# Two slots of the first expert layer with their second product split: scores there, y in the second layer

## The chip, the cores and the metric

One core of a Trainium2 chip runs the whole program. The metric is the device time of the program in microseconds; the time before is the median of three runs.

## The reference

Three parts in a row, all in f32. A linear attention (4 batches, 8 heads, 768 steps, head size 48) makes x of 3072 tokens by 384. Then two layers with 8 experts each:

```python
# first layer: each token goes to its best expert
logits = xn @ en.T / tau
expert_idx = np.argmax(logits, axis=1)
...
h = np.maximum(x[mask] @ w1[e], 0.0)
out[mask] = gate_w[mask, None] * (h @ w2[e])
# second layer: pairs (token, expert) in falling order of score, 384 tokens for each expert
logits = x @ w_gate
order = np.argsort(-flat)
...
h = np.maximum(x[mask] @ w1[e], 0.0)
out[mask] = h @ w2[e]
```

Both layers widen 384 to 1024 and go back. The second layer cannot begin to assign before it has the scores of all tokens, and it assigns greedily: each of seven phases finds the next expert that fills up.

## The kernel before, in words

The attention sorts its rows of x by expert into `sorted_rows`. The first layer (`first_layer`, from L1257) works through slots of 128 rows of one expert; 27 are used here. In a slot `x_transposes` (L1466) turns x on TensorE, 24 matmuls of 128 columns (L1492) make the hidden layer in `p_h`, ScalarE's relu (L1379) writes `hid_t`, and 8 matmuls of 392 columns (L1503) make `p_o`: 384 columns of y, and 8 of the second layer's scores, since `w2s` carries the product of w2 and the second layer's gate beside w2. VectorE writes the scores (`logits_out`, L1439) and y times the gate (L1457); ScalarE's queue stores y in `y_rows` (L1387). The transposes of the next slot stand in the middle of the second product, ahead of its fifth matmul.

Around this ScalarE computes the norm and the exponential for the gate, with a table load ahead of each (L1366, L1383). VectorE works in the order `scale`, `gate`, `x_evac` of the next slot (L1435), `logits_out`, y. SP loads the w1 of slot i + 1 when the hidden layer of slot i - 1 is done (`load_w1`, L39); GpSimd loads the w2 of an expert when the last slot of the expert before last is done. Slots 0 to 2 are written out, the rest run in a hardware loop of two slots per pass (`loop`, L1280).

The second layer (`second_layer`, from L1529) interleaves phases and experts by an order written out by hand in TensorE's function. In phase 0 TensorE has no expert to work on yet. VectorE makes 31 candidate thresholds and compares all scores with them (`offer`, L1765), TensorE counts (`count`, 31 matmuls, L1937), VectorE looks which threshold fits, TensorE spreads the answer (`digit`, L1944); this runs four times. Then `take`, `total` (L1948), `members`, `rank` (L1953), `rows` and `tables` (L1962) give the table of the expert's tokens, `read_table` tells it, GpSimd gathers the rows of `y_rows` (`get`, L1677) and the first expert's products start (L1983, L1999). Fillers (`keep_busy`, L119) stand where TensorE would otherwise rest from `rank` on. A block of the program ends with a barrier of all engines, so one stands between the two layers.

Of the kernel before, what the change touches and what calls it, by code (L numbers as in the profile page):

```python
# [79 lines left out]
WEIGHTS_AT = 10, 11, 16, 17  # L80
QUAD, HF = 4, FF // 2
# [8 lines left out]
def shared(nc, sb, ps, sem, io, keep):  # L90

    for name, shape, kind in (("ident", [P, P], F32), ("mask", [P, P], F32), ("tri", [P, P], BF16),
# [16 lines left out]
                              ("hid_t", [P, KF, P], F32), ("y_row", [P, 2, HD], F32)):  # L109
# [86 lines left out]
def attention(nc, general, sb, ps, sem, io, keep):  # L196
# [40 lines left out]
    w2t = sb("w2t", [P, QUAD, KD, HF], F32)  # L237
# [779 lines left out]
def attention_any(nc, sb, ps, sem, io, keep):  # L1017
# [15 lines left out]
    s_turn = sem("z_turn")  # L1033
# [208 lines left out]
FIRST = ("init", "expert", "turn", "xt", "xtev", "h", "relu", "o", "y", "lgdone", "gate", "ssq", "root", "arg", "exp")  # L1242
# [14 lines left out]
def first_layer(nc, sb, ps, sem, io, keep):  # L1257
    ident = keep["ident"]
    slot_row, slot_expert, last_slot = (keep[n] for n in ("slot_row", "slot_expert", "last_slot"))
    logits, tokens = keep["placed"]  # L1260
    w1s, w2s, s_w, s_slot, s_pads = (keep[n] for n in ("w1s", "w2s", "s_w", "s_slot", "s_pads"))
# [11 lines left out]
    (s_init, s_expert, s_turn, s_xt, s_xtev, s_h, s_relu, s_o, s_y, s_lgdone, s_gate, s_ssq, s_root, s_arg, s_exp,  # L1273
# [3 lines left out]
    SURE = (NT - AHEAD - 1 + 1) // 2  # L1277
    PAIRS = (SLOTS + AHEAD - 3) // 2

    def loop(eng, body):  # L1280

        for i in range(AHEAD + 1):
            body(i, i % 2, i // 2)
        eng.wait_ge(s_plan, SLOT_STEPS)
        used = eng.value_load(last_slot[0:1, E - 1:E], min_val=NT, max_val=SLOTS + AHEAD)
        with eng.Fori(0, SURE) as j:
            body(2 * j + 3, 1, j + 1)
            body(2 * j + 4, 0, j + 2)

        def further(j):  # L1290


            if j < PAIRS:
                with eng.If(used > 2 * j + 3):
                    body(2 * j + 3, 1, j + 1)
                    body(2 * j + 4, 0, j + 2)
                    further(j + 1)
        further(SURE)
        return eng.snap((used // 2) * 2)
# [5 lines left out]
    def is_slot(i, n):  # L1305
        return isinstance(i, int) and i == n

    with nc.Block() as block:
        @block.sync
        def _(sp):  # L1310
# [11 lines left out]
            last = loop(sp, body)  # L1322
            sp.sem_inc(s_init, 1)
            for k in range(2):
                sp.wait_ge(s_slot[k], 16 + 8 * last)
                sp.sem_inc(s_init, 1)
# [22 lines left out]
        def _(act):  # L1349
# [18 lines left out]
            def body(i, q, turn):  # L1368
# [6 lines left out]
                for g in range(0 if is_slot(i, 0) else 2):  # L1375
# [3 lines left out]
                    act.activation(hid_t[:, half * g:half * (g + 1), :], p_h[g][:, :, :], ACT.Relu).then_inc(s_relu, 1)  # L1379
# [6 lines left out]
                act.wait_ge(s_y, i + 1 + CREDIT)  # L1386
                act.dma_start(io["y_rows"][bass.ds(place(i, shifted) * P, P), :], y_row[:, q, :]).then_inc(s_out[q], 16)  # L1387
# [6 lines left out]
            act.sem_inc(s_init, 1)  # L1394

        @block.vector
        def _(dve):
# [47 lines left out]
            def body(i, q, turn):  # L1445
# [9 lines left out]
                logits_out(i, q)  # L1455
                dve.wait_ge(s_out[q], 16 * turn + CREDIT)
# [8 lines left out]
        def _(pe):  # L1465
# [7 lines left out]
            def body(i, q, turn):  # L1473
# [55 lines left out]
def second_layer(nc, general, sb, ps, sem, io, keep):  # L1529
# [63 lines left out]
    w1s, w2s = keep["w1s"], keep["w2s"]  # L1593

# [35 lines left out]
    s_stored = sem("b_stored", False)  # L1630

# [16 lines left out]
    with nc.Block() as block:  # L1648
# [19 lines left out]
        def _(pool):  # L1668
# [21 lines left out]
            pool.wait_ge(s_stored, 1)  # L1690
            get(0)
# [8 lines left out]
        def _(act):  # L1700
# [15 lines left out]
            act.sem_inc(s_stored, 1)  # L1716
            for i in range(TE):
                x_evac(0, i)
# [207 lines left out]
        def _(pe):  # L1926
# [76 lines left out]

            pe.wait_ge(s_v, HIGH)
# [498 lines left out]
```

## Time and profile before

| what | value |
|---|---|
| three runs, us | 828.15, 829.2, 829.27 |
| profiled execution, us | 820.85 |
| its span, us | 819.1 |
| mean granted TensorE clock in it | 0.984 of 2.4 GHz |
| TensorE busy | 779.0 us, 95% |
| VectorE, ScalarE, GpSimd busy | 53%, 39%, 18% |
| first layer's slots, from the profile | 198 to 484 us |
| first search of the second layer | 486 to 515 us |

Times inside the program are read on the profiled execution's scale, from the first instruction of its span. Busy shares are averages over stages with different limits. In the rows an f32 matmul shows as two records and a bf16 one as one; transposes show as one.

### The profile page before, as it was taken

What the parts mean: (1) busy time and instruction counts of PE and PEld (TensorE: products, weight loads), DVE (VectorE), ACT (ScalarE), POOL (GpSimd) and SP (SyncE); (2) the same over time, 40 slices, a digit from 0 to 9 for tenths busy, and PEclk for the clock granted to TensorE, in tenths of its full rate; (3) what the DMA queues carried; (4) which work ended last, traced back from release to release, by engine and by line L of the source; (5) the groups of instructions that cost most, each with busy time, mean ns of one, the idle gap of its engine ahead of it and who ended that gap; (6) DMA issues with size and microseconds to landing.
All of it is one profiled execution on the core that took longest, in us unless ns stands there. A gap on an engine that the chain in (4) does not pass through costs nothing. (4 is left out here: it accounts for less than half of the span.)

```text
span 819.1 us, 17097 instructions
## 1 busy us (share of the span) xinstructions
PE 779.0 (95%) x6003; PEld 562.7 (69%) x6004; DVE 436.7 (53%) x1194; ACT 322.5 (39%) x818; POOL 149.6 (18%) x151
## 2 busy tenths in 40 slices
PE   8999999997999999999999964899999999999996
PEld 7778777876777788887777854655666565655653
DVE  8989898944332232333323348466757677673000
ACT  4878787853444444444444420112121211112120
POOL 5114343430000000000000000106232240402201
PEclk9999999999999999999999995999999999999999
DMA  8879899625667565667575421332515052446100
GB/s 282 310 262 354 312 352 320 237 74 191 221 258 246 204 201 198 221 230 262 183 267 179 163 77 59 126 128 76 183 39 194 22 192 89 143 150 216 50 10 32
DMA packets 68856, 149.71 MB, mean 183 GB/s; under 512 B 4968, under 2 KB 37104, under 8 KB 68784
## 3 DMA queue, kind: packets, MB, share of 16 engines
q1 hardware_dynamic: 53952, 114.03, 39.2%
q0 software_dynamic: 6912, 23.75, 8.5%
q10 hardware_dynamic: 7920, 10.99, 4.1%
q8 instruction: 43, 0.70, 0.4%
q14 instruction: 29, 0.24, 0.1%
HBM read 130.06 MB, written 18.69 MB: 182 GB/s over the span
## 5 line engine op out<-in xcount | busy, mean ns | idle before, releaser
L1503 PE MATMUL p_o<-w2s,hid_t 128*128 (+1 forms) x432 | 152.7, 497 | 0.0
L1492 PEld LDWEIGHTS p_h<-x_t,w1s 128*128 128x128 f32 x1248 | 143.4, 192 | 7.2
L1492 PE MATMUL p_h<-x_t,w1s 128*128 128x128 f32 x1248 | 143.5, 275 | 0.0
L1983 PE MATMUL p_gh<-g_t,w1s 128*128 128x384 f32 x384 | 132.8, 494 | 0.0
L1999 PE MATMUL p_go<-w2s,g_hid 128*128 128x384 f32 x384 | 131.5, 489 | 0.0
L1503 PEld LDWEIGHTS p_o<-w2s,hid_t 128*128 128x128 f32 x432 | 78.7, 192 | 46.3 <-issue 1.8
L1983 PEld LDWEIGHTS p_gh<-g_t,w1s 128*128 128x128 f32 x384 | 70.0, 190 | 45.7 <-issue 6.1
L1999 PEld LDWEIGHTS p_go<-w2s,g_hid 128*128 128x128 f32 x384 | 70.3, 190 | 42.1
L1379 ACT ACTIVATE hid_t<-p_h 128x512 f32<-128x512 f32 x52 | 31.0, 597 | 155.4 <-PE p_h L1492 146.4
L1722 ACT ACTIVATE g_hid<-p_gh 128x384 f32<-128x384 f32 x64 | 31.4, 490 | 113.0 <-PE p_gh L1983 113.0
L1429 DVE TENSOR_SCALAR col<-col 128x1 f32<-128x1 f32 x27 | 4.1, 154 | 131.2 <-ACT ex L1383 131.2
L1677 POOL DMA_INDIRECT g_in<-y_rows,table x24 | 29.2, 1217 | 244.7 <-DVE table L1842 239.9
L1687 POOL DMA_INDIRECT out<-o_row,table x24 | 44.3, 1846 | 80.4 <-ACT o_row L1710 44.8
L1772 DVE TENSOR_TENSOR reach<-free_best,cand 128x3968 bf16<-128x3968 f32 (+2 forms) x19 | 58.6, 3084 | 0.7
L518 ACT ACTIVATE diag_v<-v_pad,diag 128x48 f32<-128x48 f32 x192 | 48.0, 327 | 0.0
L467 POOL TENSOR_TENSOR r_dec<-kr_t,decays 128x512 f32<-128x512 f32 x24 | 28.6, 1192 | 103.2 <-issue 60.4
L1710 ACT ACTIVATE o_row<-p_go 128x384 f32<-128x384 f32 x24 | 11.8, 490 | 87.7 <-PE p_go L1999 87.7
L1703 ACT ACTIVATE g_t<-p_gx 128x384 f32<-128x384 f32 x22 | 10.8, 490 | 70.5 <-PE p_gx L1970 70.5
L1383 ACT ACT_TABLE_LOAD x27 | 34.6, 1283 | 3.7 <-issue 3.2
L1339 POOL COPY w2s<-w2g 128x64 f32<-128x64 f32 x6 | 1.4, 237 | 185.7 <-PE p_o L1503 185.7
L1834 DVE TENSOR_TENSOR row_is<-row_b,iota_p 128x2048 bf16<-128x2048 bf16 (+1 forms) x16 | 34.9, 2221 | 0.3
L1366 ACT ACT_TABLE_LOAD x27 | 34.6, 1283 | 0.5
(269 smaller groups left out, 1052.2 us busy)
## 6 DMA issues: line engine op xcount, KB each, us to landing
w1s<-in_w SPq DMA_DIRECT2D x28, 1536.0 KB, 6.3
kr_t<-in_kr_t SPq DMA_DIRECT2D x24, 512.0 KB, 5.7
w2t<-in_w_t SPq DMA_DIRECT2D x16, 768.0 KB, 7.9
w1s<-in_w1b SPq DMA_DIRECT2D x8, 1536.0 KB, 6.4
w2s<-in_w2b SPq DMA_DIRECT2D x8, 1536.0 KB, 10.0
w2s<-in_w POOLq DMA_DIRECT2D x12, 768.0 KB, 6.4
w_pad<-in_w_t SPq DMA_DIRECT2D x24, 256.0 KB, 6.0
v_pad<-in_v_pad SPq DMA_DIRECT2D x24, 256.0 KB, 8.2
```

Of the source, the lines that this page charges most:

```text
L518: ins = act.activation(diag_v[:, t % 2, h, :], v_pad[:, q, h, 0:D], ACT.Copy, scale=diag[:, t % 2, h:h + 1])
L1366: act.activation(col[:, q, 0:1], col[:, q, 15:16], ACT.Sqrt).then_inc(s_root, 1)
L1379: act.activation(hid_t[:, half * g:half * (g + 1), :], p_h[g][:, :, :], ACT.Relu).then_inc(s_relu, 1)
L1383: act.activation(ex[:, :], lg[:, q, :], ACT.Exp, bias=col[:, q, 9:10], accum_out=col[:, q, 10:11]).then_inc(s_exp, 1)
L1492: ins = pe.matmul(p_h[g][:, m, :], w1s[:, q, a, f:f + P], x_t[:, q, a, :], start=(a == 0), stop=(a == KD - 1))
L1503: ins = pe.matmul(p_o[:, :], hid_t[:, m, :], w2s[:, bass.ds(half, 1), m, :].rearrange("p o n -> p (o n)"), start=(m == 0), stop=(m == KF - 1))
L1687: pool.indirect_dma_start(out=io["out"][:, :], out_offset=place(1, p, i), in_=o_row[:, p % 2, i, :], in_offset=None).then_inc(s_out[p % 2] ...
L1722: act.activation(hid[:, m, :], p_h[(KF * p + m) % 3][:, :], ACT.Relu).then_inc(s_relu, 1)
L1772: dve.tensor_tensor(reach(n)[:, at, :], free(p)[:, at].unsqueeze(2).broadcast_to([P, len(part), n]), cand[:, 0:n].unsqueeze(1).broadcast_t ...
L1834: dve.tensor_tensor(row_is[:, at, :], row_b[:, 1, at].unsqueeze(2).broadcast_to([P, size, P]), iota_p[:, :].unsqueeze(1).broadcast_to([P, ...
L1983: ins = pe.matmul(p_h[n % 3][:, :], w1s[:, p % 2, a, m * P:(m + 1) * P], x_t[:, a, :], start=(a == 0), stop=(a == KD - 1))
L1999: ins = pe.matmul(p_o[n % 2][:, :], hid[:, m, i * P:(i + 1) * P], w2s[:, p % 2, m, 0:HD], start=(m == 0), stop=(m == KF - 1))
```

## The change

The slots 3 and 4 (`LATE`) are late slots. There the second product takes only the 8 score columns of `w2s`, the next slot's transposes stand ahead of it, the relu writes `hid_late`, VectorE keeps the gate in `gate_late` in place of writing y, and no y is stored. SP loads the late slots' w2 into `w2_late` (room that the attention used for `w2t`), once after the third and once after the sixth pass of its loop. In the second layer's phase 0 TensorE makes the two y's with 16 matmuls of 384 columns (`late`), in groups between the steps of the search; ScalarE multiplies by the gate and stores, and GpSimd's first gather waits for both stores. Six of the ten fillers after `rank` and one between the halves of `tables` go. One more pair of slots is written out, and the loop has one pass less. A semaphore is saved by reusing another (`s_init`, `z_turn`).

```diff
+LATE = AHEAD + 1, AHEAD + 2
...
+                              ("gate_late", [P, len(LATE)], F32)):
         keep[name] = sb(name, shape, kind)
 
...
     wg, w2g = keep["wg"], keep["w2g"]
-    w2t = sb("w2t", [P, QUAD, KD, HF], F32)
...
-    SURE = (NT - AHEAD - 1 + 1) // 2
-    PAIRS = (SLOTS + AHEAD - 3) // 2
+    FIXED = LATE[-1] + 1
+    SURE = (NT - FIXED + 1) // 2
+    PAIRS = (SLOTS + AHEAD - FIXED) // 2
+
+    def loop(eng, body, between=None):
+        for i in range(FIXED):
             body(i, i % 2, i // 2)
...
-        with eng.Fori(0, SURE) as j:
-            body(2 * j + 3, 1, j + 1)
-            body(2 * j + 4, 0, j + 2)
+        parts = [range(0, SURE)] if between is None else [range(0, 3), range(3, 6), range(6, SURE)]
+        for n, part in enumerate(parts):
+            if n > 0:
+                between(n - 1)
+            with eng.Fori(part[0], part[-1] + 1) as j:
+                body(2 * j + FIXED, 1, j + FIXED // 2)
+                body(2 * j + FIXED + 1, 0, j + FIXED // 2 + 1)
...
+
+    def late(i):
+
+        return LATE.index(i) if isinstance(i, int) and i in LATE else None
+
+    def hidden(i):
+        return hid_t if late(i) is None else keep["hid_late"][:, late(i), :, :]
...
-            last = loop(sp, body)
-            sp.sem_inc(s_init, 1)
+
+            def load_late(k):
+                expert = sp.value_load(slot_expert[0:1, LATE[k]:LATE[k] + 1], min_val=0, max_val=E - 1)
+                sp.dma_start(w2_late[:, k, :, :], io["w2"][bass.ds(expert, 1), :, :].rearrange(
+                    "o (m p) n -> p (o m) n", p=P)).then_inc(s_w[k], 16)
+            last = loop(sp, body, load_late)
...
-                    act.activation(hid_t[:, half * g:half * (g + 1), :], p_h[g][:, :, :], ACT.Relu).then_inc(s_relu, 1)
+                    act.activation(hidden(i)[:, half * g:half * (g + 1), :], p_h[g][:, :, :], ACT.Relu).then_inc(s_relu, 1)
...
                 act.wait_ge(s_y, i + 1 + CREDIT)
+                if late(i) is not None:
+                    act.sem_inc(s_out[q], 16)
+                    return
                 act.dma_start(io["y_rows"][bass.ds(place(i, shifted) * P, P), :], y_row[:, q, :]).then_inc(s_out[q], 16)
...
                 logits_out(i, q)
+                if late(i) is not None:
+                    dve.tensor_copy(keep["gate_late"][:, late(i):late(i) + 1], col[:, q, 12:13]).then_inc(s_y, 1)
+                    return
                 dve.wait_ge(s_out[q], 16 * turn + CREDIT)
                 dve.tensor_scalar(y_row[:, q, :], p_o[:, 0:HD], col[:, q, 12:13], None, ALU.mult).then_inc(s_y, 1)
...
-                    if m == 4 and not first:
+                    if m == (4 if late(i) is None else 0) and not first:
                         x_transposes(i + 1, 1 - q, turn if q == 0 else turn + 1)
-                    ins = pe.matmul(p_o[:, :], hid_t[:, m, :],
-                                    w2s[:, bass.ds(half, 1), m, :].rearrange("p o n -> p (o n)"),
+                    of = slice(0 if late(i) is None else HD, HD + E)
+                    ins = pe.matmul(p_o[:, of], hidden(i)[:, m, :],
+                                    w2s[:, bass.ds(half, 1), m, of].rearrange("p o n -> p (o n)"),
                                     start=(m == 0), stop=(m == KF - 1))
                 ins.then_inc(s_o, 1)
...
             pool.wait_ge(s_stored, 1)
+            pool.wait_ge(s_late_stored, 16 * len(LATE))
             get(0)
...
+            shifted = act.value_load(keep["shift"][0:1, 0:1], min_val=0, max_val=AHEAD)
+            for k, i in enumerate(LATE):
+                act.wait_ge(s_late, k + 1)
+                act.activation(y_late[:, k, :], p_o[k][:, :], ACT.Copy, scale=keep["gate_late"][:, k:k + 1]
+                               ).then_inc(s_late_out, 1)
+                act.wait_ge(s_late_out, k + 1)
+                act.dma_start(io["y_rows"][bass.ds((i - shifted) * P, P), :], y_late[:, k, :]
+                              ).then_inc(s_late_stored, 16)
...
+                if p == 0 and i > 0:
+                    pe.wait_ge(s_late_out, i)
...
+            def late(k, blocks):
+
+                for m in blocks:
+                    if m == 0:
+                        pe.wait_ge(keep["s_w"][k], 32)
+                    ins = pe.matmul(p_o[k][:, :], keep["hid_late"][:, k, m, :], w2_late[:, k, m, :],
+                                    start=(m == 0), stop=(m == KF - 1))
+                    if m == KF - 1:
+                        ins.then_inc(s_late, 1)
+
+            late(0, range(0, 1))
             pe.wait_ge(s_v, HIGH)
             pe.transpose(p_m[0:1, :], high[:, :], ident[:, :]).then_inc(s_bound, 1)
             pe.wait_ge(s_v, BOUND)
             pe.matmul(p_m[:, 0:1], ones[0:1, :], bound[0:1, :], start=True, stop=True).then_inc(s_bound, 1)
-            for k in range(len(FAR)):
-                count(0, k)
-                digit(0, k)
+            late(0, range(1, 4))
+            count(0, 0)
+            digit(0, 0)
+            late(0, range(4, 6))
+            count(0, 1)
+            digit(0, 1)
+            late(0, range(6, 8))
+            count(0, 2)
+            digit(0, 2)
+            late(1, range(0, 2))
+            count(0, 3)
+            digit(0, 3)
+            late(1, range(2, 3))
             total(0)
+            late(1, range(3, 5))
             rank(0)
-            keep_busy(pe, 10, p_h[2][:, 0:P], ident)
-            tables(0, 5)
+            late(1, range(5, 8))
+            keep_busy(pe, 4, p_h[2][:, 0:P], ident)
+            tables(0, 4)
             keep_busy(pe, 15, p_h[2][:, 0:P], ident)
             count(1, 0)
```

TensorE in a slot of the first layer, `first_layer`, slot 3. Before (in the loop, the same as slot 2 written out): `p_h` is the hidden layer, `p_turn` the next slot's transposed x, `p_o` y and scores. The ISA rows compute addresses.

```order
L1492 MATMUL p_h<-x_t,w1s 128x128 x24
L1495 REGISTER_ALU
L1503 ISA
L1503 MATMUL p_o<-w2s,hid_t 128x392
...
L1470 MATMUL p_turn<-ident,x_in 128x128 x3
L1503 ISA
L1503 MATMUL p_o<-w2s,hid_t 128x392
```

And now:

```order
L1520 MATMUL p_h<-x_t,w1s 128x128 x24
L1523 REGISTER_ALU
L1498 MATMUL p_turn<-ident,x_in 128x128 x3
L1532 ISA
L1532 MATMUL p_o<-w2s,hid_late 128x8
...
L1507 TENSOR_LOAD slot_expert
```

The second product has 8 columns in place of 392, and the transposes have moved from its middle to its front.

TensorE in the first search of the second layer. Before (`p_search` holds counts and answers, `p_rows` the maximum, ranks and tables, `p_gh` the fillers' target):

```order
L2005 MATMUL p_rows<-ident,high 1x128
L2007 MATMUL p_rows<-bound,ones 128x1
L1937 MATMUL p_search<-takers,reach 31x8 x31
L1944 MATMUL p_search<-hit,ones_bf 128x1
...
L1948 MATMUL p_search<-taken_now,ones_bf 128x248
L1953 MATMUL p_rows<-member,tri 128x31
L1954 MATMUL p_rows<-before,ones_bf 128x31
L122 MATMUL p_gh<-ident 128x128 x10
```

And now:

```order
L2054 MATMUL p_go<-w_late,hid_late 128x384
L2061 MATMUL p_rows<-ident,high 1x128
L2063 MATMUL p_rows<-bound,ones 128x1
L2054 MATMUL p_go<-w_late,hid_late 128x384 x3
L1980 MATMUL p_search<-takers,reach 31x8 x31
L1987 MATMUL p_search<-hit,ones_bf 128x1
L2054 MATMUL p_go<-w_late,hid_late 128x384 x2
...
L1991 MATMUL p_search<-taken_now,ones_bf 128x248
L2054 MATMUL p_go<-w_late,hid_late 128x384 x2
L1996 MATMUL p_rows<-member,tri 128x31
L1997 MATMUL p_rows<-before,ones_bf 128x31
L2054 MATMUL p_go<-w_late,hid_late 128x384 x3
```

One late matmul has come ahead of the maximum, three ahead of the first count, two ahead of each later count, one and two around the total and three behind the rank, where four fillers are left.

## Rows read from the trace of the kernel before

**Rows 1.** Timeline, slot 3: start us, us, engine, line, op, tiles, idle before

```profile
226.19 2.80 PE L1503 MATMUL p_o<-w2s,hid_t 128*128 x8
...
227.00 1.28 ACT L1383 ACT_TABLE_LOAD   x1
...
228.72 0.15 DVE L1429 TENSOR_SCALAR col<-col 128x1 f32<-128x1 f32 x1 [4.90 <-ACT ex L1383]
...
229.74 0.56 DVE L1437 COPY x_t<-p_turn 128x384 f32<-128x384 f32 x1
...
231.78 5.52 PE L1492 MATMUL p_h<-x_t,w1s 128*128 128x128 f32 x48
```

**Rows 2.** Windows: us, then PE, PEld, DVE, ACT, POOL busy, clock, DMA share, GB/s

```profile
491.00:506.00 15.00, 5.80 (x129) 4.40 (x129) 11.57 (x44) 0.00 (x0) 0.00 (x0) 0.50 0.00 1
506.00:511.40 5.40, 3.94 (x23) 3.75 (x23) 4.91 (x14) 0.00 (x0) 0.00 (x0) 0.71 0.50 176
```

**Rows 3.** Windows of one microsecond, PE alone: busy, clock, DMA share, GB/s

```profile
488.00:489.00 1.00, 0.34 (x2) 0.82 0.00 0
...
509.00:510.00 1.00, 1.00 (x9) 0.94 0.72 266
```

**Rows 4.** Timeline, end of the first layer and first search

```profile
481.15 2.80 PE L1503 MATMUL p_o<-w2s,hid_t 128*128 x8
...
486.53 0.42 DVE L1846 SCALAR_TENSOR_TENSOR at_best<-logits 128x248 f32<-128x248 f32 x1 [1.62 <-PEq L1308]
...
488.66 0.58 PE L2007 MATMUL p_rows<-bound,ones 1*128 1x1 f32 x2 [0.94 <-DVE bound L1854]
...
491.18 1.12 PE L1937 MATMUL p_search<-takers,reach 128*31 128x8 bf16 x31 [1.94 <-DVE reach L1772]
...
492.51 0.15 DVE L1780 TENSOR_TENSOR filled<-p_search,room 31x8 f32<-31x8 f32 x1
...
492.91 0.18 PE L1944 MATMUL p_search<-hit,ones_bf 31*128 31x1 bf16 x1 [0.61 <-DVE hit L1781]
...
494.51 1.12 PE L1937 MATMUL p_search<-takers,reach 128*31 128x8 bf16 x31 [1.42 <-DVE reach L1772]
...
503.78 0.60 PE L1948 MATMUL p_search<-taken_now,ones_bf 128*128 128x248 bf16 x1 [1.10 <-DVE taken_now L1788]
...
506.15 0.21 PE L1953 MATMUL p_rows<-member,tri 128*128 128x31 bf16 x1 [1.77 <-DVEq L1888]
```

**Rows 5.** Timeline, from the rank to the first gather

```profile
506.23 3.85 PE L122 MATMUL p_gh<-ident 128*128 128x128 f32 x20
...
507.29 0.39 SPq L1656 DMA_DIRECT2D w1s<-in_w1b  x1
...
513.86 3.59 PE L122 MATMUL p_gh<-ident 128*128 128x128 f32 x30
...
515.44 1.03 POOL L1677 DMA_INDIRECT g_in<-y_rows,table  x1 [101.07 <-DVE table L1842]
```

**Rows 6.** Timeline of PE, short products in the attention

```profile
121.08 0.83 PE L875 MATMUL p_route<-enT,x_tr 128*128 128x8 f32 x6
121.78 0.63 PE L919 MATMUL p_kb<-ident,k_dec 128*128 128x128 f32 x4
```

**Rows 7.** Groups of the page: count, busy us, mean ns, idle before

```profile
L1492 PEld LDWEIGHTS p_h<-x_t,w1s 128*128 128x128 f32 x1248 | 143.4, 192 | 7.2
```

**Rows 8.** Line L1356, the 26 loads of x: from issue to landing

```profile
DMA to landing us min/median/max: 2.3/2.4/5.1
```

**Rows 9.** DMA issues of the page: count, KB each, median us to landing

```profile
w1s<-in_w SPq DMA_DIRECT2D x28, 1536.0 KB, 6.3
```

**Rows 10.** Chain that ended last: start us, us, what (total, second product)

```profile
541.28 0.45 PE p_search L1948
...
581.84 5.16 PE p_go L1999 x16
```

**Rows 11.** Line L1387, the 27 stores of y: from issue to landing

```profile
DMA to landing us min/median/max: 1.8/2.0/7.0
```

More of the change, by code:

```diff
@@ L236, in attention @@
     wg, w2g = keep["wg"], keep["w2g"]
-    w2t = sb("w2t", [P, QUAD, KD, HF], F32)
+    w2t = keep["w2_late"][:, :].rearrange("p (j a f) -> p j a f", j=QUAD, a=KD)
     w2g_t = sb("w2g_t", [P, HF], F32)
@@ L1032, in attention_any @@
     s_k = sem("z_const")
-    s_turn = sem("z_turn")
+    s_turn = keep["first"]["turn"]
     s_in = sem("z_in")
@@ L1239, in route_any @@
     return {"sync": on_sync, "gpsimd": on_gpsimd, "vector": on_vector, "tensor": on_tensor}
-FIRST = ("init", "expert", "turn", "xt", "xtev", "h", "relu", "o", "y", "lgdone", "gate", "ssq", "root", "arg", "exp")
+FIRST = ("expert", "turn", "xt", "xtev", "h", "relu", "o", "y", "lgdone", "gate", "ssq", "root", "arg", "exp")
 FIRST_PAIRS = ("xin", "xfree", "out")
@@ L1260, in first_layer @@
     logits, tokens = keep["placed"]
+    w2_late = keep["w2_late"][:, :].rearrange("p (k m n) -> p k m n", k=len(LATE), m=KF)
     w1s, w2s, s_w, s_slot, s_pads = (keep[n] for n in ("w1s", "w2s", "s_w", "s_slot", "s_pads"))
@@ L1276, in first_layer @@
     SCALE, GATE = 9, 13
-    SURE = (NT - AHEAD - 1 + 1) // 2
-    PAIRS = (SLOTS + AHEAD - 3) // 2
-    def loop(eng, body):
-        for i in range(AHEAD + 1):
+    FIXED = LATE[-1] + 1
[3 more added lines that the diff above has]
+        for i in range(FIXED):
             body(i, i % 2, i // 2)
@@ L1285, in loop @@
         used = eng.value_load(last_slot[0:1, E - 1:E], min_val=NT, max_val=SLOTS + AHEAD)
-        with eng.Fori(0, SURE) as j:
-            body(2 * j + 3, 1, j + 1)
-            body(2 * j + 4, 0, j + 2)
+        parts = [range(0, SURE)] if between is None else [range(0, 3), range(3, 6), range(6, SURE)]
[5 more added lines that the diff above has]
+                body(2 * j + FIXED + 1, 0, j + FIXED // 2 + 1)
         def further(j):
             if j < PAIRS:
-                with eng.If(used > 2 * j + 3):
-                    body(2 * j + 3, 1, j + 1)
-                    body(2 * j + 4, 0, j + 2)
+                with eng.If(used > 2 * j + FIXED):
+                    body(2 * j + FIXED, 1, j + FIXED // 2)
+                    body(2 * j + FIXED + 1, 0, j + FIXED // 2 + 1)
                     further(j + 1)
@@ L1393, in _ @@
             act.wait_ge(s_xin[1], 16 + 8 * last + CREDIT)
-            act.sem_inc(s_init, 1)
+            act.sem_inc(s_turn, 1)
         @block.vector
@@ L1593, in second_layer @@
     w1s, w2s = keep["w1s"], keep["w2s"]
+    y_late = sb("y_late", [P, len(LATE), HD], F32)
+    w2_late = keep["w2_late"][:, :].rearrange("p (k m n) -> p k m n", k=len(LATE), m=KF)
     p_s = ps("p_search", [P, E + 2 + E * SLOTS])
@@ L1630, in second_layer @@
     s_stored = sem("b_stored", False)
+    s_late = sem("b_late", False)
+    s_late_out = sem("b_late_out", False)
+    s_late_stored = sem("b_late_stored", False)
     def rows_out(eng):
```

8 lines of the change are left out of this document (5 added, 3 removed).

## The prediction

> **What bounds the kernel now.** I went from the clock and the windows to the two places that the diff touches, a slot of the first layer and the first search of the second layer, and read each as a timeline. The sums are made against the profiled execution, 819.1 us of span inside 820.85 us. The three plain runs have a median of 829.2 us, 8.35 us more. I take differences from the profile and subtract them from 829.2, which assumes that the extra 8.35 us lie in neither place.
>
> In the first layer TensorE never rests. Slot 3 shows it [rows 1]: its second product begins at 226.19 (8 records are 4 matmuls, since an f32 matmul leaves two records), and the next slot's first product begins at 231.78, 5.59 us later. The same 10.95 or 10.96 us stand between the starts of all slots from the second on. Under that lies a second chain which is hidden today: after the last relu ScalarE loads a table at 227.00, VectorE's gate starts at 228.72, and the copy of the next slot's transposed x, which the next product needs, runs from 229.74 to 230.30 [rows 1].
>
> In the search it is the other way round. TensorE is 5.80 us busy in the 15 us from 491 to 506, at half clock [rows 2], and VectorE's chain sets the time. The granted clock is 0.82 in the microsecond from 488 and 0.94 in the one from 509 [rows 3]. So it falls to 1.2 GHz about 4.9 us after the last product of the first layer (481.15 + 2.80 = 483.95 [rows 4]) and comes back about 3 us after the fillers that start at 506.23 [rows 5].
>
> **Part 1: the late slots, a saving.** Slots 3 and 4 multiply 8 columns of w2s instead of 392. A full matmul costs 5.3 us / 8 = 0.66 there. The nearest short one is the attention's 128x8 product: 6 records from 121.08 to 121.78, 0.233 us for each f32 matmul, bound by its weight loads [rows 6]. So 8 of them take 1.87 us instead of 5.28: TensorE gets 3.4 us per slot. It cannot use all of it. The x copy ends 230.30 - 226.19 = 4.11 us after the second product begins, and with 0.2 us for the signal and one weight load (0.19 [rows 7]) the next product starts at 4.31, not 5.59. That is **1.28 us per slot, 2.56 in all**. The bounds are 0.9 (the short product or the next x is late too) and 3.4 (VectorE's chain doesn't count).
>
> The transposes move from the middle of the second product to its start, 2.6 us earlier. They need the next slot's x, whose load landed in 2.3 to 5.1 us [rows 8]. Even one that comes 1.5 us into the second product ends in front of the gate's last step, so I charge nothing. The multiply of y (VectorE) and the y store (ScalarE's queue) go from these slots; they were beside TensorE's work. Two more slots written out instead of looped cost nothing that the profile shows: slot 2, written out, follows the same period as the looped ones.
>
> **Part 2: two more weight loads.** SP issues 1536 KB twice, each right behind a w1s load of the same size, which lands in 6.3 us [rows 9]. Two in a row land in at most 12.6. The w1s load is first in the queue, and the next one has a full slot and a half (5.6 + 5.4 + 5.6 = 16.6 us from issue to need). Nothing on SP waits behind them but the next w1s load, which is issued a slot later. Charged at nothing; if x's own load is pushed past 5.1 us twice, it could be 0.9 us.
>
> **Part 3: 16 matmuls in the gaps, a cost that hangs on the clock.** A 128x384 matmul takes 5.16 / 8 = 0.645 us at 2.4 GHz [rows 10]. At 1.2 GHz no row shows one. Its bounds are twice that, 1.29, and 1.03, by the fillers, whose 20 records took 3.85 us at the low clock and 30 took 3.59 at the high one, a factor of 1.6 [rows 5]. I take 1.29, because 384 columns outweigh the weight load more than 128 do.
> - The first matmul sits ahead of the transpose of the maximum. VectorE starts at 486.53 after the barrier [rows 4]; TensorE is free at the same time and done near 487.2, when VectorE's maximum is not yet ready. Nothing.
> - Three follow the small product of 488.66 + 0.58 = 489.24. At 2.4 GHz they end at 491.18, exactly where the first count starts: nothing. At 1.2 GHz they end at 493.1.
> - Two stand between an answer (492.91 + 0.18 = 493.09) and the next count (494.51): a gap of 1.42 us for 1.29, the same ahead of the second, third and fourth count. One goes ahead of the total (503.78), two between the total's end at 504.38 and 506.15, a gap of 1.77, and three more take the place of six fillers [rows 4, 5]. All fit at 2.4 GHz.
>
> Which clock? One matmul of 0.65 us in the idle 5 us is little, so I expect the clock to fall as before. But the three dense ones then fill TensorE from 489.24, like the fillers from 506.23 which brought the clock back in 3 us. Until 492.2 they do 3.0 / 1.29 = 2.3 matmuls, the rest takes 0.45 us: 492.7. The count adds 1.1, and VectorE, which went on at 492.51 [rows 4], goes on at 493.8: **1.3 us late**. From there on the clock is full, where it was at half before. The total took 0.60 us at the low clock and 0.45 at the high one [rows 10]; with some 0.1 us of each of the three later counts (an estimate from that pair) I take **0.5 us back**.
>
> One row speaks for the return, the fillers of rows 5; one against it, the search from 491 to 506, in which TensorE worked 5.80 of 15 us and the clock stayed at half throughout [rows 2]. The late matmuls lie between the two. If they act like the fillers the part costs 0.8 us, if like the search 6.2 (the second rival). The Trainium skill (TensorE: Matmul & The Clock Gate, What's actually happening) says that the throttled clock is the default and that activity releases it; by that rule it would be the 0.8, and the trace agrees at the fillers but not in the search.
>
> **Part 4: the late stores.** The gather at 515.44 [rows 5] must now wait for the two late y stores. The last late matmul ends near 506.4 + 1.9 = 508.3; with a ScalarE copy of 0.5 and 0.3 to issue, the store starts at 509.1. y stores landed in 1.8 to 7.0 us, median 2.0 [rows 11]: 510.9 to 516.1. The phase's w1s load, issued at 507.29, shares the engines until about 513.5 [rows 5]. Most likely it is down before 514.6, some 0.8 in front of the gather, where the table is told: nothing, up to 1.5.
>
> **Sum:** -2.56 + 1.3 - 0.5 = -1.8 us, so **827.4 us**.
>
> **Rivals.**
> - *The clock does not fall*, because the first matmul and the three dense ones leave too short a rest (18%). For it: the rest shrinks from over 7 us of near idleness to about 5. Against it: 4.9 us sufficed before. Then the search loses nothing and gains 0.5: 829.2 - 2.6 - 0.5 = 826.1.
> - *The clock falls and stays down through the search* (13%, the slower side). Place: the gaps of phase 0. Then three gaps of 1.42 us hold 2.58, 1.16 late each; the block of three costs 1.75 after VectorE's slack of 0.2; the two behind the total 0.8 and the one ahead of it 0.2: 6.2 us. 829.2 - 2.6 + 6.2 = 832.8. It decides from the point where the clock is still 0.50 at the second count; more than 2.5 us lost is a loss over all. For it: each count and each answer still leaves TensorE idle for some 0.5 us. Against it: with the added matmuls TensorE rests far less than in rows 2.
> - *The late store holds the gather* (10%): 1.5 us on the forecast, 828.9.
> - *The slot follows TensorE alone* (5%): 2 x 3.4 saved, 829.2 - 6.8 + 0.8 = 823.2. Against it the x copy of rows 1.
> - *The first layer gives less than it says* (12%): x or the added loads come late in and around the late slots, 1.3 saved in place of 2.56: 828.7.
>
> **The numbers.** The forecast holds 42%; its own range is 826.5 to 828.9 (the clock back at once, or one stretch later). About 0.2%, 1.66 us, is what a measurement can tell from no change, so faster means under 827.5. That is 0.25 of the forecast's 0.42, the full clock and the TensorE case: 0.48. Slower, over 830.9, is the low clock and 0.02 of late stores: 0.15. The rest is 0.37. The range leaves out the TensorE case and the low clock, together 0.18, and reaches from the full-clock case with its bound to a clock that returns halfway: 825.6 to 830.6.
>
> **What would show it.** In the late slots the next product should start 4.3 us after the second begins, with the idle time ended by the x copy. The layer's last product should end near 481.4 on the profile's scale. In the search: the clock at 0.50 for one stretch of 3 to 5 us and then 1.00, the first count about 1.5 us later against the small product, the later gaps of 1.4 unchanged, and the gather released by the table and not by a store. I am wrong if the search is longer by over 2.5 us, or if a late slot's saving is not near 1.3.

## The result, and the profile after

| what | before | after |
|---|---|---|
| median, us | 828.46 (20 runs) | 832.06 (20 runs) |
| profiled execution, its span, us | 820.85, 819.1 | 829.61, 827.8 |
| mean granted TensorE clock | 0.984 | 0.978 |
| TensorE busy, us | 779.0 | 790.3 |

The ratio after to before is **1.004, 95% interval 1.0029 to 1.0051**: some 3.3 us slower (2.4 to 4.2). I had forecast 827.4 us, faster than before, with a range up to 830.6. The forecast was wrong in direction and in range.

The page of the profile after, its span and busy times:

```profile
span 827.8 us, 17095 instructions
...
PE 790.3 (95%) x6021; PEld 569.9 (69%) x6022; DVE 435.9 (53%) x1194; ACT 323.6 (39%) x820; POOL 145.3 (18%) x151
```

TensorE is busy 11.3 us longer. Some 3 us of that are new work: the two short products (1.85 to 1.98 us each) come on top of the moved columns, and seven fillers go. For the rest the same kind of work takes it longer: that is a first sign of the clock.

**Where the time went, by stages.** A slot's period runs from the start of its first product to that of the next. The first layer is taken from the start of slot 1's first product to the end of its last product, the search from VectorE's first step to the first gather.

| stage, us | before | after |
|---|---|---|
| periods of slots 3, 4, 5 | 10.95, 10.96, 10.96 | 9.57, 11.12, 13.69 |
| first layer | 285.84 | 286.85 |
| search | 28.91 | 31.97 |
| first gather to the second layer's first product | 8.67 | 7.51 |
| second layer's first product to the end | 295.0 | 298.1 |

The three slots lost 1.5 us where 2.56 were to be won, and the search lost 3.1 us. The last row is not laid to the change: over all kernels of this study it lies between 293.2 and 298.8 us, and it was 297.5 in one without a late slot. Nor is the period of slot 1, which is 10.96 to 12.56 us in kernels with and without the change, nor the time ahead of it (slot 1's first product starts at 198.11 before, at 200.78 after, and at 202.68 in e8, a kernel without a late slot), nor the row above the last, 6.97 to 9.04 us. They differ from one profiled execution to the next, so below only slots 3 to 5, the search and the timed ratio are compared.

**The first layer after.** Timeline of TensorE from 219 to 262 us (start, length, engine, line, operation, tiles, idle before; the counterpart of [rows 1]):

```profile
222.97 5.52 PE L1520 MATMUL p_h<-x_t,w1s 128*128 128x128 f32 x48
230.20 0.52 PE L1498 MATMUL p_turn<-ident,x_in 128*128 128x128 f32 x3 [1.72 <-DMA x_in<-sorted_rows]
230.56 1.98 PE L1532 MATMUL p_o<-w2s,hid_late 128*128 x16
232.54 7.02 PE L1520 MATMUL p_h<-x_t,w1s 128*128 128x128 f32 x48
239.41 0.49 PE L1498 MATMUL p_turn<-ident,x_in 128*128 128x128 f32 x3
239.73 1.85 PE L1532 MATMUL p_o<-w2s,hid_late 128*128 x16
243.66 8.25 PE L1520 MATMUL p_h<-x_t,w1s 128*128 128x128 f32 x48 [2.07 <-DVE x_t L1462]
```

Slot 3 is 222.97 to 232.54, slot 4 is 232.54 to 243.66. The short products take 1.98 and 1.85 us, as forecast (1.87). But the first products behind them, the same 48 records, take 7.02 and 8.25 us and not 5.52. The same stretch in windows of one microsecond, TensorE alone (total, busy, granted clock, share and rate of the DMA engines):

```profile
229.00:230.00 1.00, 0.00 (x0) 1.00 0.89 184
...
232.00:233.00 1.00, 0.99 (x6) 0.57 1.00 414
233.00:234.00 1.00, 1.00 (x7) 0.50 1.04 430
...
236.00:237.00 1.00, 1.00 (x11) 1.00 0.81 284
...
242.00:243.00 1.00, 0.00 (x0) 0.69 0.97 385
...
246.00:247.00 1.00, 1.00 (x6) 0.50 0.55 141
...
249.00:250.00 1.00, 1.00 (x10) 0.90 0.00 0
```

In each late slot the engine waits 1.7 or 2.1 us and works 1.9 us on 8-column matmuls, and each time the granted clock falls to 0.50 (1.2 GHz). It is back at 1.00 by 236 in slot 4, some 3 us into the next first product. In slot 5 it comes back only in the microsecond from 249, of which it spends 0.2 at the low clock (0.90): 5.5 us in. That explains the periods: -1.38 in slot 3; +0.16 in slot 4, which is -1.34 and +1.50 (7.02 against 5.52); +2.73 in slot 5 (8.25 against 5.52).

**The search after**, timeline from 490 us on (counterpart of [rows 4]):

```profile
490.24 0.42 DVE L1889 SCALAR_TENSOR_TENSOR at_best<-logits 128x248 f32<-128x248 f32 x1 [1.64 <-PEq L1325]
...
492.36 0.58 PE L2063 MATMUL p_rows<-bound,ones 1*128 1x1 f32 x2 [0.94 <-DVE bound L1897]
...
492.87 4.21 PE L2054 MATMUL p_go<-w_late,hid_late 128*128 128x384 f32 x6
...
497.01 0.99 PE L1980 MATMUL p_search<-takers,reach 128*31 128x8 bf16 x31
...
498.62 2.93 PE L2054 MATMUL p_go<-w_late,hid_late 128*128 128x384 f32 x4
...
501.48 0.96 PE L1980 MATMUL p_search<-takers,reach 128*31 128x8 bf16 x31
...
503.04 1.56 PE L2054 MATMUL p_go<-w_late,hid_late 128*128 128x384 f32 x4
...
504.53 1.09 PE L1980 MATMUL p_search<-takers,reach 128*31 128x8 bf16 x31
```

The three late matmuls take 4.21 us, and the first count starts 4.65 us after the small product, where it was 2.52 before (488.66 to 491.18 [rows 4]): 2.1 us. The next two take 2.93 us, and from the first count to the second there are 4.47 us (497.01 to 501.48) for 3.33 before: 1.1. The two after them take 1.56 us, and from the second count to the third there are 3.05 for 3.22 before: 0.2 back. The stretches behind that are within 0.04 us of those of before.

There is a third fall, outside these rows. In all ten kernels here that have the late matmuls the clock falls once more, in nine of them at the products for the tables, where the change took fillers away: after, TensorE rests 2.11 us ahead of them (1.32 before) and the clock is at 0.50 from 518.9 to 522.3. The gather comes no later by it, since VectorE's steps set its time. But the fillers behind it run longer, and the next phase's first count waits for them.

### The profile page after: what moved, and what is told of

Its sections match the earlier page's. It is cut to its first block and busy times, and to the rows that moved or that the text cites. A ratio compares the mean times of both kernels' runs of the same rounds, so it can differ in the third digit from the quotient of the medians.

```text
span 827.8 us, 17095 instructions
## 1 busy us (share of the span) xinstructions
PE 790.3 (95%) x6021; PEld 569.9 (69%) x6022; DVE 435.9 (53%) x1194; ACT 323.6 (39%) x820; POOL 145.3 (18%) x151
## 3 DMA queue, kind: packets, MB, share of 16 engines
q10 hardware_dynamic: 7920, 10.99, 4.0%
## 5 line engine op out<-in xcount | busy, mean ns | idle before, releaser
L1520 PEld LDWEIGHTS p_h<-x_t,w1s 128*128 128x128 f32 x1248 | 147.3, 196 | 8.9 <-issue 2.2
L1520 PE MATMUL p_h<-x_t,w1s 128*128 128x128 f32 x1248 | 147.8, 280 | 2.1 <-DVE x_t L1462 2.1
L1532 PE MATMUL p_o<-w2s,hid_t 128*128 (+1 forms) x400 | 142.2, 499 | 0.0
L1532 PEld LDWEIGHTS p_o<-w2s,hid_t 128*128 128x128 f32 x400 | 73.5, 194 | 43.3 <-issue 2.4
L1401 ACT ACTIVATE hid_t<-p_h 128x512 f32<-128x512 f32 x48 | 28.7, 597 | 145.5 <-PE p_h L1520 145.5
L1721 POOL DMA_INDIRECT out<-o_row,table x24 | 39.9, 1664 | 79.5 <-ACT o_row L1745 44.5
L481 POOL DMA_INDIRECT sorted_rows<-rows,pos x24 | 30.2, 1259 | 19.2 <-DVE rows L727 11.6
```

Of the source, the lines that this page charges most:

```text
L1520: ins = pe.matmul(p_h[g][:, m, :], w1s[:, q, a, f:f + P], x_t[:, q, a, :], start=(a == 0), stop=(a == KD - 1))
L1532: ins = pe.matmul(p_o[:, of], hidden(i)[:, m, :], w2s[:, bass.ds(half, 1), m, of].rearrange("p o n -> p (o n)"), start=(m == 0), stop=(m = ...
L1721: pool.indirect_dma_start(out=io["out"][:, :], out_offset=place(1, p, i), in_=o_row[:, p % 2, i, :], in_offset=None).then_inc(s_out[p % 2] ...
```

## The experiments

My theory (A in the expectations) was: **the clock makes the whole loss, in both places.** A late slot gives TensorE's time back as idle time, the clock falls, and the next full product pays more than the slot saved; in the search the matmuls run at the low clock. The rivals were that late loads of x or w2, the earlier transposes, or the written-out slots cost it. Each ratio is to runs of the kernel before on the same chip. "Slots" is the sum of the periods of slots 3 to 5, 32.87 us before.

| kernel | slots, us | search, us | ratio, 95% |
|---|---|---|---|
| the change | 34.38 | 31.97 | 1.004, 1.0029 to 1.0051 |
| e0, the change again | 34.92 | 30.68 | 1.0037, 1.0021 to 1.0054 |
| e1, first layer's part alone | 34.81 | 28.91 | 1.0023, 1.0003 to 1.0044 |
| e2, search's part alone | 32.87 | 30.89 | 1.0014, 1.0 to 1.0029 |
| e3, fillers behind the short product | 35.61 | 30.06 | 1.0016, 0.9992 to 1.0041 |
| e4, x copy ahead of the gate | 33.89 | 31.94 | 1.0014, 0.9998 to 1.003 |
| e5, fillers ahead of the transposes | 30.32 | 30.69 | 0.9982, 0.9964 to 1.0 |
| e6, e5 and fillers at the barrier | 30.32 | 28.87 | 0.9937, 0.9918 to 0.9955 |
| e6b, the same again | 30.32 | 28.83 | 0.9955, 0.9933 to 0.9976 |
| e7, e2 and fillers at the barrier | 32.87 | 29.17 | 0.9989, 0.9975 to 1.0002 |
| e8, before with fillers in the search | 32.87 | 30.09 | 1.0007, 0.999 to 1.0024 |
| e9, transposes back in the middle | 34.87 | 31.99 | 1.0032, 1.0018 to 1.0046 |

**First layer alone.** The late slots give their scores; the second layer is as before. The y of two slots is left out.

```diff
-            last = loop(sp, body, load_late)
+            last = loop(sp, body)
...
-            late(0, range(1, 4))
+            for k in range(len(FAR)):
+                count(0, k)
+                digit(0, k)
```

> The first-layer half of the change alone: slots 3 and 4 make only their scores, the second layer is as before, the two w2 loads are left out, and the y rows of the two slots are left out of the computation (a stale y_row is stored in their place). Theory A, the clock falls in the late slots: TensorE's clock drops to 1.2 GHz around slots 4 and 5, the three slots from 3 to 5 take 33 to 35 us instead of 32.9, and the kernel is 0 to 2 us slower than before. Theory B, the loss is all in the search: the slots save 1.28 us each and the kernel is 2.6 us faster.

Timeline of its TensorE:

```profile
231.54 0.52 PE L1495 MATMUL p_turn<-ident,x_in 128*128 128x128 f32 x3 [1.68 <-DMA x_in<-sorted_rows]
...
234.38 8.08 PE L1517 MATMUL p_h<-x_t,w1s 128*128 128x128 f32 x48
...
246.55 7.17 PE L1517 MATMUL p_h<-x_t,w1s 128*128 128x128 f32 x48 [2.07 <-DVE x_t L1459]
```

The two slow first products stand here without any late load of w2, so the added loads do not make them. Nor do the late matmuls: the search is 28.91 us, as before. TensorE has 2 x 3.4 us less to do, and the slots take 1.9 us more.

**Search alone.** Slots 3 and 4 make and store their whole y, and the second layer makes it again.

```diff
-                    if m == (4 if late(i) is None else 0) and not first:
+                    if m == 4 and not first:
...
-                    of = slice(0 if late(i) is None else HD, HD + E)
+                    of = slice(0, HD + E)
```

> The second-layer half alone: slots 3 and 4 make and store their whole y in the first layer as before, and the same y is made once more by the 16 matmuls in the gaps of the search, with both w2 loads and both late stores. Theory A: 2 to 3 us slower than before, from late matmuls at 1.2 GHz ahead of the first two counts; the first layer keeps 10.96 us for each slot. Theory B: over 5 us slower, since this half must hold the whole loss and the 2.6 us that the first layer saves.

The search loses 2.0 us with a first layer that is as before. Slots 3 and 4 are written out here as in the change, their relu writes `hid_late`, and they keep 10.95 and 10.96 us: being written out costs them nothing. The search:

```profile
492.31 3.92 PE L2050 MATMUL p_go<-w_late,hid_late 128*128 128x384 f32 x6
496.16 0.93 PE L1976 MATMUL p_search<-takers,reach 128*31 128x8 bf16 x31
...
497.69 1.56 PE L2050 MATMUL p_go<-w_late,hid_late 128*128 128x384 f32 x4
```

The block of three takes 3.92 us, the next two 1.56: the clock is back one gap earlier than in the profile of the change. The parts' excesses, 0.0023 and 0.0014, add up to the 0.0037 of the change measured again. Their intervals (0.0003 to 0.0044 and 0 to 0.0029) are too wide for that to exclude a third cost; it shows only that none is needed.

> The change as it is, for a second trace on the chip of the three runs beside it. Both theories: 2 to 4 us slower than before. Theory A, the clock falls in the late slots and around the first late matmuls: the first layer from its first looped product to its end takes 1 to 2 us more than before, and the search from VectorE's first step to the first gather 2 to 3 us more than 28.9.

The change again, on the chip of e5 to e9: the slots take 10.07, 12.22 and 12.63 us, the search 30.68. How the loss is shared between the places varies; the timed loss is the same within its interval.

**Fillers behind the short product.** Nine matmuls of the identity follow it.

```diff
                 ins.then_inc(s_o, 1)
+                if late(i) is not None:
+                    keep_busy(pe, 9, p_spare[:, :], ident)
```

> The change with nine fillers of 128x128 behind the short product of each late slot, into a PSUM bank of their own, so that TensorE works until the next x is there. Theory A: the clock stays at 2.4 GHz, slots 3 to 5 take about 30.3 us, and the kernel is 3 to 4 us faster than the change without them. Theory B: no difference, or slower by the fillers' overhang.

```profile
228.00:229.00 1.00, 0.92 (x6) 0.66 0.85 213
```

```profile
228.08 0.67 PE L1499 MATMUL p_turn<-ident,x_in 128*128 128x128 f32 x3 [2.02 <-DMA x_in<-sorted_rows]
...
231.82 3.83 PE L125 MATMUL p_spare<-ident 128*128 128x128 f32 x18
...
242.88 2.25 PE L125 MATMUL p_spare<-ident 128*128 128x128 f32 x18
245.10 5.62 PE L1521 MATMUL p_h<-x_t,w1s 128*128 128x128 f32 x48
```

A miss that taught the place. In slot 3 the wait is ahead of the transposes, not behind the product: x is waited for there. The first row is the window of TensorE from 228: at 0.66 it holds 0.7 us of low clock, so the clock fell near 228.3, 0.2 us into the transposes and ahead of the short product. A rest of 2.02 us behind a full first product was enough by itself. The fillers came after that, where TensorE had nothing to wait for; they ran in 3.83 us in place of 2.25 and delayed the next product, a period of 14.95 us. In slot 4, where the wait stands behind the short product, they fill it: the period is 9.61 and the next first product takes 5.62 us. The short product between them did not lower the clock. One kernel holds both answers: filler behind the wait costs, filler in the wait gives the slot's whole saving.

**The copy of x earlier.** VectorE copies the next x ahead of the gate in the late slots.

```diff
+                if late(i) is not None:
+                    x_evac(i + 1, 1 - q)
                 gate(i, q)
```

> The change with VectorE's copy of the next x ahead of the gate in the late slots. If the chain of table load, gate and copy bounds a late slot, as the forecast says, the next product starts some 2 us earlier, TensorE rests less and the clock falls less: 2 to 6 us faster than the change. If the load of x bounds it (TensorE waited 1.7 us for it in slot 3), slot 3 gains under 1 us and slot 4 about 2 us.

```profile
230.30 0.52 PE L1500 MATMUL p_turn<-ident,x_in 128*128 128x128 f32 x3 [1.67 <-DMA x_in<-sorted_rows]
...
241.58 0.56 DVE L1462 COPY x_t<-p_turn 128x384 f32<-128x384 f32 x1 [6.32 <-PE p_turn L1500]
...
244.31 7.25 PE L1522 MATMUL p_h<-x_t,w1s 128*128 128x128 f32 x48 [1.08 <-issue]
```

The slots take 9.83, 11.38 and 12.68 us, 1.0 lost: taking a wait away gave little. Slot 3 waits for the load of x, which no copy can precede. In slot 4 the copy ended at 242.14 and the product started at 244.31, with 1.08 us of "issue" ahead of it: TensorE waited for nothing that the profile shows. This is where the written-out slots end and the loop begins; whether the entry into the loop takes the time was not tested. The clock fell all the same (7.25 us).

**Transposes back in the middle of the second product**, the rest as in the change.

```diff
-                    if m == (4 if late(i) is None else 0) and not first:
+                    if m == 4 and not first:
```

> The change with the transposes of the next x back in the middle of the late slot's short product, and no fillers. If the wait for x at the front of the product is what lowers the clock, four short products run ahead of it, slot 3 keeps the clock and the first layer is 2 us shorter than in the change. If the short products hold the clock no better than rest does, TensorE's dense work is just as little and the first layer is within 1 us of the change.

```profile
231.45 0.52 PE L1498 MATMUL p_turn<-ident,x_in 128*128 128x128 f32 x3 [0.71 <-issue]
...
234.00 7.22 PE L1520 MATMUL p_h<-x_t,w1s 128*128 128x128 f32 x48 [1.24 <-DVE x_t L1462]
...
245.32 8.54 PE L1520 MATMUL p_h<-x_t,w1s 128*128 128x128 f32 x48 [2.06 <-DVE x_t L1462]
```

The wait for x becomes 0.71 us of "issue" and 1.24 of waiting for its copy, and the slots lose 2.0 us: the move of the transposes is not the cause. Wherever the rest lies in the slot, the first product behind it pays.

**Fillers ahead of the transposes**, in the wait for x.

```diff
+                    if m == 0 and late(i) is not None:
+                        keep_busy(pe, 9, p_spare[:, :], ident)
```

> The change with nine fillers in each late slot ahead of the transposes of the next x, where TensorE waited 1.7 to 2.0 us for the load of x in slot 3. Theory A: the clock stays at 2.4 GHz, the starts of the first products after slots 3 and 4 are 9.6 to 9.8 us apart, slot 5 keeps 10.96, and the first layer is 2.3 to 2.6 us shorter than before, against 1 to 2 longer in the change; in time 3 to 4 us faster than the change. Theory B, the x load and not the clock costs the late slots: the fillers change nothing in them.

The slots take 9.58, 9.68 and 11.06 us: -2.55 in all, against a forecast of -2.56. The search keeps its loss (30.69), and the ratio falls from 1.0037 to 0.9982. No work or load was taken from the change; 18 useless matmuls were added where TensorE rested, and nothing else. That the two numbers agree so closely owes something to the count of nine: the copy of x ends at 230.48 in slot 3 and the filled TensorE at 230.54, so either would have set the period.

**Both places held.** Besides, six fillers behind the first layer's last product and three behind the transpose of the maximum.

```diff
+            keep_busy(pe, 6, p_spare[:, :], ident)
...
+            keep_busy(pe, 3, p_h[2][:, 0:P], ident)
             pe.wait_ge(s_v, BOUND)
```

> As the run with nine fillers ahead of the transposes, and six fillers behind the first layer's last product and three behind the transpose of the maximum, so that TensorE rests little on both sides of the barrier. Theory A: the clock does not fall in the search either, the search takes 28.5 to 28.9 us to the first gather, and the kernel is 5 us faster than the change and 2 to 3 us faster than before. If the rest in the barrier is still enough to lower the clock, the search takes 30 to 31 us and only the first layer's gain is left.

> The same kernel as the run that holds the clock at both places, once more, since its time (5.2 us under before) is better than its stages explain (2.6 us in the first layer, nothing in the search). If the stages are right, 2 to 4 us faster than before; if something else in it gains, again over 5.

Of the second of these two, TensorE in the first layer; then all engines from slot 3's second product to the end of slot 4, and around the barrier, with clock, DMA share and rate last:

```profile
227.45 2.17 PE L125 MATMUL p_spare<-ident 128*128 128x128 f32 x18
229.49 0.55 PE L1499 MATMUL p_turn<-ident,x_in 128*128 128x128 f32 x3
229.87 1.85 PE L1535 MATMUL p_o<-w2s,hid_late 128*128 x16
231.67 5.60 PE L1521 MATMUL p_h<-x_t,w1s 128*128 128x128 f32 x48
```

```profile
227.00:242.00 15.00, 14.94 (x133) 14.78 (x132) 4.60 (x25) 9.13 (x17) 0.78 (x1) 1.00 0.81 286
...
484.00:491.00 7.00, 5.41 (x49) 3.30 (x48) 5.32 (x15) 0.00 (x0) 0.00 (x0) 1.00 0.08 30
```

The clock is 1.00 in both stretches, with the DMA engines busy to 0.81 in the first. After, with 0.71, it was 0.87 in the counterpart of the first, and 0.56 from 243 to 250, in slot 5's first product:

```profile
228.00:243.00 15.00, 11.86 (x91) 11.54 (x89) 3.73 (x23) 8.21 (x16) 0.78 (x1) 0.87 0.71 246
```

And its search:

```profile
487.40 0.38 PE L2068 MATMUL p_rows<-bound,ones 1*128 1x1 f32 x2 [0.27 <-DVE bound L1901]
487.70 2.20 PE L2058 MATMUL p_go<-w_late,hid_late 128*128 128x384 f32 x6
489.92 1.09 PE L1984 MATMUL p_search<-takers,reach 128*31 128x8 bf16 x31
...
491.75 1.56 PE L2058 MATMUL p_go<-w_late,hid_late 128*128 128x384 f32 x4
```

The three late matmuls take 2.20 us, the first count starts 2.52 us after the small product, exactly as before, and the search takes 28.83 us against 28.91. The 16 matmuls cost nothing. The kernel is **faster than before in both measurements, 0.9937 (0.9918 to 0.9955) and 0.9955 (0.9933 to 0.9976)**. That is 5.2 and 3.7 us. The slots and the search explain 2.6 of them; the first interval, 3.7 to 6.7 us, lies above that, the second, 2.0 to 5.5, holds it. Whether the rest is real, and in which stage, stays open. From the first gather to the second layer's first product these traces have 7.07 and 7.86 us for 8.67 before, but the two kernels with the second layer's old order of work (e1 and e8) have 7.56 and 7.38 too, so the trace of before may have been a long one there.

"Held" is also too much for the third place. The 30 fillers behind the tables:

```profile
512.50 5.14 PE L125 MATMUL p_gh<-ident 128*128 128x128 f32 x30
```

They took 3.59 us before [rows 5]. The clock was at 0.50 from 512.3 to 515.8 in e6b, behind a rest of 2.11 us, and from 513.1 to 516.5 in e6. The count behind them started 3.5 us after the gather in e6b, 2.7 in e6 and the change, and 4.65 in e5, against 2.6 before, and from the fillers to the first product TensorE has no wait in e5 and e6b. From the gather to that product these two take 9.04 and 7.86 us, where the shortest trace has 6.97, so an estimate of what this place can cost is 0.9 to 2 us. No run here fills it.

**The search's part with fillers at the barrier**, first layer whole (e2 with the two lines above):

> The second-layer half alone (slots 3 and 4 whole in the first layer, their y made once more in the gaps) with the same fillers at the barrier. Theory A: the search takes 28.5 to 28.9 us against 30.9 without these fillers, and the kernel equals before within 1 us. Otherwise the 16 matmuls cost their 2 us at the high clock too.

The search takes 29.17 us in place of 30.89: the loss there was the clock. The ratio agrees, 0.9989 (0.9975 to 1.0002) in place of 1.0014 (1.0 to 1.0029), though the intervals touch. It is not clear of 1, so the search's part shows no gain of its own: the gain has to come from the slots.

**Fillers in the search of the kernel before**, no late slot at all, for the rival that the fillers gain by themselves:

```diff
+            keep_busy(pe, 9, p_h[2][:, 0:P], ident)
             count(0, 0)
...
+                keep_busy(pe, 6 if k < 3 else 3, p_h[2][:, 0:P], ident)
```

> The kernel before, with no late slot, but with fillers of 128x128 at the barrier (six and three) and in the gaps of the first search (nine, six, six, six, three, six) so that its clock is held there too. If the fillers by themselves make the gain, it is 2 us or more faster than before. Theory A expects the search to be only 0 to 0.6 us shorter, and the time within 1 us of before, so that the gain of the run with both clocks held belongs to the late slots.

```profile
491.52 0.27 PE L2007 MATMUL p_rows<-ident,high 128*1 128x128 f32 x1 [2.16 <-DVE high L1852]
...
493.20 3.70 PE L122 MATMUL p_gh<-ident 128*128 128x128 f32 x18
```

No gain: 1.0007 (0.999 to 1.0024). But it is a weaker answer than meant. TensorE still rested 2.16 us ahead of the maximum's transpose, where the late kernels have their first matmul, the clock fell (18 records in 3.70 us), and the search took 30.09 us. So it shows that fillers strewn into this kernel don't bring e6's gain, not what it would do with the clock held throughout.

## Why the prediction was wrong

- **Part 1, the saving of a late slot: the term was right, and one was missing.** The short product takes 1.85 us (forecast 1.87), and 1.28 us a slot is what the periods show once the clock holds (2.55 for 2.56, in e5, e6 and e6b). In slot 4 after, the next product starts 4.25 us after the transposes that now open the second product (239.41 to 243.66), released by the copy of x as forecast, where I had 4.31. The failed step is that "TensorE gets 3.4 us per slot" was read as harmless spare time: the 2 us that it cannot use were charged at nothing. It cost 1.50 + 2.73 us in the profile after, so the slots gave +1.5 in place of -2.56. I asked how TensorE loses its clock only for the search. The profile before shows two falls, there and ahead of slot 1 (191 to 195, behind a rest of 4.19 us). The longest rest in it that left the clock at 1.00 is 1.85 us (up to 12.27, in the attention). So it could not have told that 2 us are enough, but it did not tell the opposite either, and no rival of mine had it. I had stated as a test that "a late slot's saving is not near 1.3" would prove me wrong; it did, with a period of 13.69 us in the full slot behind.
- **"I charge nothing" for x.** The load of x landed in 2.3 to 5.4 us after, 2.3 to 5.1 before [rows 8]. In slot 3 it took 4.5 us for 3.3 before, and TensorE waited 1.7 us for it, ahead of the transposes. In length I was right, since the period is 9.57 us even so; but that wait is the rest behind which the clock falls.
- **Part 2, two loads: right.** The slots around them keep 10.95 to 10.99 us.
- **Part 3, the search: the mechanism right, the size not.** The clock fell as said (before, it did so 4.7 us behind the layer's last product and not 4.9: 0.82 leaves 0.36 us at the low clock up to 489), and at the low clock a late matmul took 1.40 us (4.21 / 3) where I had 1.29. I had +1.3 - 0.5. The profile after has +2.1 for the block of three, +1.1 for the two behind it and 0.2 back, 3.1; e0 has +2.1 and 0.3 back, 1.8. The 0.5 back was too much: counts went from 1.12 to 1.09 us at full clock, and the total stayed at 0.60, so the pair of [rows 10] didn't show the clock's share. The failed step here is the clock's return within the block of three, 3 us after its start, which I took from the fillers of [rows 5] and which made the block 3.45 us long. It took 4.21 us after and in e0, 3.92 in e2. Counted from the block's start the clock came back after 3.5 us in e2, 4.4 in e0 and, with a count and an answer in between, 8.9 in the profile after:

```profile
491.00:492.00 1.00, 0.39 (x2) 0.77 0.00 0
...
501.00:502.00 1.00, 1.00 (x21) 0.61 0.00 0
502.00:503.00 1.00, 0.50 (x19) 1.00 0.00 0
```

  That is about halfway to my second rival ("stays down through the search", +6.2). I had named a search longer by over 2.5 us as what would make me wrong. The Trainium skill (TensorE: Matmul & The Clock Gate, What's actually happening) says that the point at which the clock changes depends on where in a free-running window the work lands and so varies from run to run. The traces agree that it varies: the second block of late matmuls took 2.93 us after, and 1.56 us in e0, the same kernel.
- **Part 4, the stores: right.** The first late y is stored long before; the second is issued at 516.02, 0.2 us behind the forecast's 509.1 moved by the 6.7 us by which the rank is later. It took 5.2 us to land, so it was down at 521.2, just as the table was told (521.15 + 0.17), and the profile puts the gather at 522.21 down to the table:

```profile
516.02 0.34 ACTq L1758 DMA_DIRECT2D y_rows<-y_late  x1
...
522.21 1.03 POOL L1711 DMA_INDIRECT g_in<-y_rows,table  x1 [104.14 <-DVE table L1885]
```

  It was right by 0.1 us only. In e5 the profile names the store and not the table as what released the gather, but the gather comes 1.05 us behind the table's step there too, as it does elsewhere: it cost nothing.
- **The sum.** Forecast -2.56 + 1.3 - 0.5 = -1.8. Measured in the profile after: +1.5 and +3.1, 4.6; in e0 +2.05 and +1.8, 3.8; by the timed ratio 2.4 to 4.2. The chances gave 0.15 to slower, by a single case in the search. Most of the miss is the slots: 4.1 us, against 2.3 in the search. A late slot that loses more than it saves was none of my rivals: "the first layer gives less than it says" stopped at 1.3 saved.

## What to carry to other kernels

Work taken from TensorE inside a stage where it never rested is not worth its duration: first ask whether the next thing it waits for comes earlier too, and if not, read the clock of the full product behind the rest. If work has to be moved from a dense stage into a sparse one, fill both the gap it leaves and the gap ahead of the place it goes to; here 18 + 9 useless matmuls turned 1.0037 into 0.9937 and 0.9955. Put the filler in front of the instruction that waits, and look up in the trace which one that is, since it differs from slot to slot: in slot 3 filler ahead of the wait gave a period of 9.58 us, filler behind it 14.95. And look again once the fillers are in: here a third fall was left.

## What the runs showed of the hardware

- **A rest of 2 us can be enough to lose the clock.** 1.72 us of rest and 1.98 us of 8-column matmuls were followed by a granted clock of 0.57 and 0.50, as were 1.85 us of them and 2.07 us of rest; in e3 a rest of 2.02 us behind a full product was enough alone. Neither is enough every time: in the kernel before a rest of 1.85 us (up to 12.27) left the clock at 1.00, and in e6b the same 1.85 us of short products did, behind 2.17 us of 128-column fillers. Behind the first layer's last product, with at most a few short matmuls in between, the clock fell after 4.7 us before, 3.9 after, 2.8 in e0 and 2.1 in e2: the time it takes is not the same in every execution.
- **With most of it at the low clock** a product of 48 records of 128 columns, f32, took up to 8.54 us (e9) in place of 5.52, and a 128x384 f32 matmul 1.40 us in place of 0.73 (4.21 / 3 and 2.20 / 3).
- **Where the written-out slots end and the loop begins** TensorE stood 1.08 us in "issue" in e4, behind 2.2 us of transposes and short products. At the same place in e5, behind 4.2 us of work with the fillers, it did not. The cause was not tested.
- **A load of 198 KB** landed in 2.3 to 5.4 us here: the median of 2.5 us says little of the one that is waited for. What made some of them slow was not tested.
